# Linear-attention query features: transposed products on TensorE against sketched factors spread by DMAs

## The reference

```python
# layer 1: attention with sketched features, r = 8
def phi(x):
    a = np.einsum('rd,bhsd->bhsr', S1, x)
    b = np.einsum('rd,bhsd->bhsr', S2, x)
    return np.einsum('bhsi,bhsj->bhsij', a, b).reshape(*x.shape[:-1], r * r)
q_p, k_p = (phi(q), phi(k))
kv = np.einsum('bhsf,bhsd->bhfd', k_p, v)
z = np.sum(k_p, axis=2)
num = np.einsum('bhsf,bhfd->bhsd', q_p, kv)
den = np.einsum('bhsf,bhf->bhs', q_p, z)[..., None] + 1e-06
x = num / den                                  # heads side by side: 128 channels
# layer 2: u = x + real(fft over tokens and channels), normalised, 128 -> 512 -> 128
u = x + mixed
ch = np.maximum(un @ w_ch1, 0.0) @ w_ch2
x = u + ch
# layer 3: 128 -> 1024, convolution of 3 taps over tokens, gate, 1024 -> 128
h = np.maximum(x @ w_in, 0.0)
gate = 1.0 / (1.0 + np.exp(-conv_out))
out = h * gate @ w_out
```

## Time and profile before

| | us |
|---|---|
| median of 3 runs | 276.6 |
| runs | 279.46, 276.60, 275.37 |
| the profiled execution's own time | 278.21 |
| its span, first to last instruction | 276.4 |
| PE busy in it | 254.7 |
| DVE busy | 219.1 |
| ACT busy | 186.5 |
| POOL busy | 36.2 |
| data moved by DMA | 13.04 MB |

### The profile page before, as it was taken

One profiled execution on the slowest core, in us unless ns is written; L12 is line 12 of the kernel. 1 busy time (PEld: TensorE's weight loads), 2 busy tenths in 40 slices (PEclk: granted clock), 3 DMA queues, 4 the chain that ended last, 5 costly groups with the idle time before them and its releaser, 6 DMA issues.

```text
span 276.4 us, 4299 instructions
## 1 busy us (share of the span) xinstructions
PE 254.7 (92%) x1524; PEld 211.6 (77%) x1524; DVE 219.1 (79%) x384; ACT 186.5 (67%) x353; POOL 36.2 (13%) x90
## 2 busy tenths in 40 slices
PE   8799999989889999979887999999999999999955
PEld 7789999889778888868675777677677777777633
DVE  0746879877887677756686987958699999999993
ACT  2351426234466656648969889796999799999933
POOL 0000000003321233330270740000000000000000
PEclk9999999999999999979999999999999999999999
DMA  6859620200000000000000000000100010001002
GB/s 220 321 209 365 239 90 0 89 4 0 2 0 2 1 1 2 0 1 4 0 0 0 2 0 0 0 4 0 81 0 2 0 81 0 1 4 81 0 0 81
DMA packets 4197, 13.04 MB, mean 47 GB/s; under 512 B 720, under 2 KB 1488, under 8 KB 4176
## 3 DMA queue, kind: packets, MB, share of 16 engines
q1 hardware_dynamic: 4176, 12.77, 12.6%
HBM read 10.54 MB, written 2.23 MB: 46 GB/s over the span
## 4 chain that ended last, share of the span: by engine, by line
PE 45%; DVE 30%; ACT 15%; issue 5%; DMA 2%; POOL 1%; SPq 0%; ACTq 0%; DVEq 0%; POOLq 0%
DVE arena L969 8%; DVE arena L957 8%; DVE arena L962 8%; PE ps L540 7%; PE ps L458 5%; PE ps L451 5%; PE ps L375 5%; ACT arena L662 5%; PE ps L460 4%; PE ps L459 4%; PE ps L416 4%; PE ps L387 4%; ACT arena L749 3%; ACT arena L736 3%; DMA arena<-qT_d 2%
## 5 line engine op out<-in xcount | busy, mean ns | idle before, releaser
L540 PE MATMUL ps<-arena,wout 128*128 128x364 f32 (+1 forms) x192 | 63.8, 471 | 3.5 <-DVE arena L969 3.3
L540 PEld LDWEIGHTS ps<-arena,wout 128*128 128x128 f32 x192 | 35.5, 189 | 21.5 <-DVE arena L969 5.8
L957 DVE SCALAR_TENSOR_TENSOR arena<-arena,taps 128x1088 f32<-128x1088 f32 x32 | 43.5, 1359 | 6.4 <-ACT arena L744 6.4
L458 PE MATMUL ps<-x2hi,wlo 128*128 128x364 f32 x96 | 42.5, 442 | 5.9 <-ACT arena L736 4.2
L736 ACT ACTIVATE arena<-ps 128x364 f32<-128x364 f32 x96 | 40.6, 470 | 10.2 <-PE ps L460 9.9
L962 DVE SCALAR_TENSOR_TENSOR arena<-arena,taps 128x1088 f32<-128x1088 f32 x32 | 43.5, 1358 | 0.0
L969 DVE TENSOR_TENSOR arena<-arena 128x1088 f32<-128x1088 f32 (+2 forms) x36 | 41.8, 1176 | 1.5 <-ACT arena L749 1.5
L744 ACT ACTIVATE arena<-arena,taps 128x1088 f32<-128x1088 f32 x32 | 38.5, 1204 | 1.0
L749 ACT ACTIVATE arena<-arena 128x1088 f32<-128x1088 f32 x32 | 35.2, 1102 | 4.6 <-DVE arena L962 4.6
L460 PE MATMUL ps<-x2hi,whi 128*128 128x364 f32 x96 | 31.8, 332 | 0.0
L459 PE MATMUL ps<-x2lo,whi 128*128 128x364 f32 x96 | 31.7, 330 | 0.0
(11 more groups left out here) (81 smaller groups left out, 441.3 us busy)
## 6 DMA issues: line engine op xcount, KB each, us to landing
arena<-v_d SPq DMA_DIRECT2D x4, 594.0 KB, 4.2
arena<-qT_d SPq DMA_DIRECT2D x4, 545.0 KB, 7.0
arena<-kT_d SPq DMA_DIRECT2D x3, 544.5 KB, 7.0
out_d<-arena SPq DMA_DIRECT2D x3, 544.0 KB, 2.7
cos_t<-cos_d SPq DMA_DIRECT2D x1, 926.5 KB, 5.6
sin_t<-sin_d SPq DMA_DIRECT2D x1, 926.5 KB, 7.4
wraw<-w_d SPq DMA_DIRECT2D x2, 256.0 KB, 5.0
wraw<-win_d SPq DMA_DIRECT2D x1, 512.0 KB, 5.9
```

The lines of the kernel that those rows point to most:

```text
L458: pe.matmul(out, lo, rhi, start=first, stop=False)
L540: pe.matmul(ps[:, OUT_BANK + t, 0:z - a], wout[:, c, :], gate[:, i % GATES, a:z], start=(c == 0), stop=(c == C2 - 1)).then_inc(wout_done, 1)
L957: dve.scalar_tensor_tensor(out=gate[:, i % GATES, 1:S + 1], in0=h2[:, i % HIDDENS, 0:S], scalar=taps[:, i % C2, 0:1], in1=gate[:, i % GATE ...
```

## The change

Queries are no longer the weights of their sketch but its moving side. The weights are `turned_sketch`, whose 64 columns are sorted: rows 0 to 15 of the result are the a factors of heads 0 and 1, rows 16 to 31 their b factors, and rows 32 to 63 the same for heads 2 and 3. The tokens lie along the row. ACT copies this to `ab_q`. Then SP issues DMAs within SBUF: `q_a` gets each a row 8 times (one DMA from 16 rows to 128), `q_b` gets the 16 b rows 8 times (eight DMAs of 16 rows), for each of the two pairs of heads: 18 DMAs per batch. DVE multiplies `q_a` by `q_b`, which gives the features with features in rows. The transposes, their copies on ACT and `qphi` are gone. Key features are laid out in the matching order (i, head, j), in two instructions in place of one. `block_diagonal` is one product with a mask `own`. `query_features(1)` stands behind `normalise(0)`; the later ones stay ahead of `normalise`. DMA order, the order around `token_sums(0)`, `token_sums(1)`, `moments(1)`, the last folds, and `FIRST_SLOTS` (24 for 22) change too.

```diff
+Q_PIECES = [(0, 4), (4, 8), (8, 10)]
-        FIRST_SLOTS = NC1 // 2 + 2
+        FIRST_SLOTS = NC1 // 2 + 4
+            def spread_factors(b):
+                sp.wait_ge(ab_ready, sketched(q_turn, b))
+                if b >= 2:
+                    sp.wait_ge(att_done, len(AT_PIECES) * (b - 1))
+                    sp.wait_ge(qphiT_ready, 2 * (b - 1))
+                i = b % 2
+                for pair in range(2):
+                    row = 32 * pair
+                    sp.dma_start(q_a[:, i, pair], ab_q[row:row + 16, i].unsqueeze(1).broadcast_to([16, R, NQ * TQ])).then_inc(
+                        spread[i][pair], 16)
+                    for copy in range(R):
+                        sp.dma_start(q_b[copy * 16:copy * 16 + 16, i, pair], ab_q[row + 16:row + 32, i]).then_inc(spread[i][pair], 16)
...
+            sp.dma_start(turned_sketch[:], st_d).then_inc(ld_sketch, 16)
+            load_queries(0)
             sp.dma_start(sketch[:], s_d).then_inc(ld_sketch, 16)
+            load_keys(0)
+            load_keys(1)
             load_values(0)
+            load_queries(1)
+            sp.dma_start(own[:], own_d).then_inc(ld_ident, 16)
+            spread_factors(0)
...
+            def query_sketches(b, part):
...
+                pe.matmul(ps[0:H * AB, bank_kq(n), 0:(t1 - t0) * TQ], turned_sketch[:], qT[:, b % 2, t0 * TQ:t1 * TQ],
+                          start=True, stop=True).then_inc(sk_done, 1)
-            def feature_transposes(b, n):
...
                 if n == 0:
                     pe.wait_ge(kvz_ready, b + 1)
+                    pe.wait_ge(qphiT_ready, 2 * (b + 1))
-                if c == 1 and r + 1 < NR:
+                if c == 2 and r + 1 < NR:
                     normed_transposes(r + 1)
...
+            key_values(B - 1, 0, 2 * NK)
+            token_sums(0)
             fold_transposes(B - 2)
+            token_sums(1)
             for n in range(len(AT_PIECES)):
                 attend(B - 1, n)
             channel_spectra(B - 2)
+            normed_transposes(0)
             token_sums(2)
             pe.wait_ge(wlo_ready, 2)
+            for n in range(FIRST_SLOTS):
                 slot(n)
+                if n == 3:
+                    fold_transposes(B - 1)
+                if n == 5:
+                    channel_spectra(B - 1)
...
             def query_features(b):
+                i = b % 2
+                for pair in range(2):
+                    dve.wait_ge(spread[i][pair], 16 * COPIES * (b // 2 + 1))
+                    dve.tensor_tensor(q_a[:, i, pair], q_a[:, i, pair], q_b[:, i, pair], ALU.mult).then_inc(qphiT_ready, 1)
             def block_diagonal(b):
-                dve.tensor_copy(kvz[0:F, :, 0:V1], src[0:F, :, 0:V1])
-                dve.tensor_copy(kvz[F:2 * F, :, V1:2 * V1], src[F:2 * F, :, V1:2 * V1]).then_inc(kvz_ready, 1)
+                dve.tensor_tensor(kvz[:], ps[:, KV_BANK, 0:4 * V1].rearrange("p (m c) -> p m c", m=2),
+                                  own[:].unsqueeze(1).broadcast_to([128, 2, 2 * V1]), ALU.mult).then_inc(kvz_ready, 1)
...
                 block_diagonal(b)
-                query_features(b + 1)
+                if b >= 1:
+                    query_features(b + 1)
                 normalise(b)
+                if b == 0:
+                    query_features(b + 1)
                 mirror_fold(b)
```

More of the change, by code:

```diff
@@ L221, in bank_p, with sketched @@
             return 3 + n % 2 if n < NT * NI // 2 else (n - NT * NI // 2 + 3) % 5
+        k_turn, q_turn = {}, {}
+        for turns, b in ((q_turn, 0), (k_turn, 0), (k_turn, 1), (q_turn, 1), (q_turn, 2), (k_turn, 2), (q_turn, 3), (k_turn, 3)):
+            for n in range(len(K_PIECES if turns is k_turn else Q_PIECES)):
+                turns[b, n] = len(k_turn) + len(q_turn)
+        def sketched(turns, b):
+            return max(t for (batch, _), t in turns.items() if batch == b) + 1
         tr_turns, at_turns = [], []
         for b in range(B + 1):
-            if b < B:
-                tr_turns += [("features", b, n) for n in range(TR_PIECES)]
             if b >= 1:
@@ L235, in build @@
         bank_of.update({turn: 5 + n % 3 for n, turn in enumerate(at_turns)})
-        FIRST_SLOTS = NC1 // 2 + 2
+        for n in range(2):
+            bank_of["folded", B - 1, n] = bank_of["spectra", B - 1, n] = (5, 7)[n]
+        FIRST_SLOTS = NC1 // 2 + 4
         ALL_SLOTS = NC1 + 2
@@ L757, in output @@
                     act.activation(outT[:, b % 2, a:z], ps[:, OUT_BANK + t, 0:z - a], ACT.Copy).then_inc(out_ready, 1)
-            for n in range(2, FIRST_SLOTS):
+            for n in range(FIRST_SLOTS):
                 slot(n)
+                if n == 3:
+                    fold_copies(B - 1)
+                if n == 5:
+                    spectrum_copies(B - 1)
             relu(0)
@@ L941, in _ @@
             weight_low(2, 2 * D1, 2 * D1 + D2)
+            block_diagonal(B - 1)
             mixed_rows(0)
             moments(0)
-            block_diagonal(B - 1)
             mixed_rows(1)
+            normalise(B - 1)
             moments(1)
-            normalise(B - 1)
             normed_low(0)
+            slot(0)
+            slot(1)
             mirror_fold(B - 1)
             partner_fold(B - 2)
-            slot(0)
-            slot(1)
-            partner_fold(B - 1)
             def left_tap(i):
@@ L1042 @@
         sketch[h * D:(h + 1) * D, h * AB + R:(h + 1) * AB] = S2.T
+    columns = [(2 * pair + h) * AB + i for pair in range(2) for half in range(2)
+               for h, i in ([(h, i) for i in range(R) for h in range(2)] if half == 0 else
+                            [(h, R + j) for h in range(2) for j in range(R)])]
+    turned_sketch = np.ascontiguousarray(sketch[:, columns])
+    own = np.zeros((R, 2, R, 2, V1), f)
+    own[:, 0, :, 0], own[:, 1, :, 1] = 1.0, 1.0
+    own = own.reshape(128, 2 * V1)
     ident = np.eye(128, dtype=f)
```

252 lines of the change are left out of this document (120 added, 132 removed).

## The result

| | us |
|---|---|
| before, median | 277.5 (275.4 to 279.5) |
| changed, median | 341.6 (336.1 to 348.6) |
| ratio | 1.217, 95% interval 1.203 to 1.231 |

The forecast was wrong by 58 us and the range missed it. The rival of the quarter rate, with a chance of 0.20, gave 332.

What follows compares the result with a forecast made beforehand. PE and DVE together were taken to bound the attention stage, DVE the end of layer 3. Terms +1.9 +1.6 -0.7 +1.0 -0.6 +1.1 -3.4 +1.7 sum to +2.6: 280.8 for the profiled execution, 279 as median; range 270 to 300.

Steps and rivals of the forecast that it cites:

- The rival of the quarter rate: Spread DMAs from 16 SBUF rows run at 105 GB/s, 21.3 us per batch, giving 332 us; chance 0.20.
- What bounds the kernel: Attention stage: PE and DVE bound it together, PE alone only for batch 0; last part of layer 3: DVE.
- what PE saves: Transposes, query sketches and layer 3's fp32 products: at most 8.3 us together, if PE were the bound throughout.
- I take the full rate: Spreads within SBUF assumed at 419 GB/s, 5.3 us per batch, so their issue, 8.5 us, is the longer.
- the forecast held 6.9: Terms tied to spreads: 1.9 + 1.8 before batch 0's attend, 1.5 waiting for spreads 3, 1.7 for the clock.
- DVE's savings: Per batch: query features 2.40 us for 2.83, `block_diagonal` 0.25 for 0.48, key features about 0.05 more.
- batch 0 to 1: From `attend(0)` to `attend(1)`: 15.7 us where 14.1 before, +1.6 us, query features no longer running beside PE's products.
- 1 to 2: From `attend(1)` to `attend(2)`: 15.3 us where 16.0 before, -0.7 us, by a dropped DVE wait and cheaper `block_diagonal`.
- The start's 1.9: Start of the kernel: `attend(0)` at 22.5 us instead of 20.6, +1.9 us, behind the first spreads.
- Start of layer 3: -3.4: Two more slots ahead of layer 3 fill PE's pauses and avoid the clock's fall there, -3.4 us.
- -0.6: From `mixed_rows(0)` to slot 4: its first product at 87.1 to 87.2 us instead of 84.00, +3.2 in all, -0.6 here.
- Clock, +1.7: PE's new pauses ahead of `attend` of batches 0 to 2: one clock fall taken on the path, +1.7 us.

## Why the prediction was wrong

- **What bounds the kernel**: right for the kernel before. Three quarters of the transposes are worth 2 us, so what PE saves had little value.
- **"I take the full rate"** is the step that failed. I argued from a DMA share of 1.00 at 419 GB/s that the engines were what was full. Measured: 111 GB/s in the kernel (2.23 MB in 20.1 us) and 92 alone, between my own bounds of 52 and 419. The reading excluded nothing: at 105 GB/s the share is 1.00 too. What sets the rate is the groups into which the 16 source rows fall, four here. All spreads together cost 44 us, of which the forecast held 6.9 (see the version without spreads), so this step is worth about 37 of the 58 us. The Trainium skill's 104 GB/s (same page and section) agreed with what came, within 12%, and I had set it beside the sum instead of in it. The issue at 0.47 us was a second error of the same term: 0.62.
- **DVE's savings** were near: query products 2 x 1.29 us for 2.83 (I had 2.40), `block_diagonal` 0.29 for 0.48 (0.25). They vanish behind 46.1 us of waits.
- **The rival of the quarter rate** was right in its mechanism, and near in its number (332 for 337) partly by luck. Spreads 0 last from 8.0 to 30.4, where DVE's second product starts (forecast 12.4 to 33.7). Spreads 3 are issued by 100.1 and DVE has the last of them at 102.7, 10 us ahead of the forecast 113. `attend(3)` still starts at 123.0 (forecast 120.4), since the work between took 20 us for 7, from 102 to 123 us at a granted clock of 0.50.
- **Start and batches without spreads.** In the version with unused transposes `attend` starts at 23.9, 40.1, 57.6 and 72.7 us, before at 20.6, 34.7, 50.7 and 66.9. So it costs 3.4 us at the start, 2.1 more for batch 0 to 1 (forecast 1.6) and 1.4 for 1 to 2 (-0.7), and the last gives 1.0 back (+1.0). The sum, 5.8, is near the forecast 3.8, but only batch 0 to 1 came by the path that I had: PE waits 1.6 us there for DVE's `block_diagonal`. The start's 1.9 was a wait for spreads, and without them I had 18.8 for 23.9: PE's own products end last there (DVE waits 5.3 us for them), about 1.9 us of unused transposes among them.
- **"Start of layer 3: -3.4"**: wrong in sign, and the second step that failed. I took PE's two pauses for a loss that two slots would fill, "the same work at another place". The pause and the clock's fall at that place went, but at their old place the slots filled ACT's waits, and both came back later. Slots and steps together cost 10 us (ratio 1.056 to 1.020). The two slots alone cost 3.5 in the kernel before, so the order of steps is worth some 6 to 7 (an estimate, across two kernels); it had no term of its own beyond -0.6.
- **Clock, +1.7**: too small. Behind the last wait for spreads alone the half clock costs 6.6 us (22.2 for 15.6). The whole of it is open.

Sum of what was measured: 44 for the spreads, 10 for slots and steps, 6 for start and batches (slot 0 at 80.4 for 74.4), against 60 found.

## What to carry to other kernels

Before data are spread by DMAs from few rows of SBUF, count the groups of rows that they are read from: spacing the source rows cost next to nothing here, made an eightfold copy by itself 1.9 times as fast (13.1 us for 24.3) and took 18 us off the kernel. A full DMA share is no proof of full rate. And before replacing an operation, leave most of it out once: here that would have shown that three quarters of it are worth about 2 us. Last, a gap on an engine isn't free room: what fills it may have filled a larger one later.

## What the runs showed that I had not expected

- 64 neighbouring source rows are no faster than 16 at step 8 (13.0 and 13.1 us).
- Sixteen copies of 16 rows within SBUF took 0.62 us each to issue on SP, loads from HBM to as many rows 0.46.
- Without spreads PE ran at 1.2 GHz for 34 us from 58.5 us on, although busy 10.00 of 10 us from 65 to 75, while with short transposes between its products it was at 2.4 GHz there.
- A late filler was worth more than an early one here: PE's wait for the relu grew from 4.2 to 8.2 us when only two slots were taken away from layer 3.
- Two queues that read different groups reached 235 GB/s together, where one alone had 171.
